# One more copy of v, a shorter warm-up, and five pooled normalisations moved to GpSimd, in a kernel of attention and two feed-forward layers

## The chip, the cores and the metric

The kernel runs on one core of one Trainium2 chip. The metric is the device time in microseconds (us) of one execution; the kernel before took 814.86 us in the median of three runs (814.63 to 815.61). The core has four compute engines that run side by side and wait for one another through semaphores: TensorE (PE in the profile; its weight loads are listed as PEld), VectorE (DVE), ScalarE (ACT) and GpSimd (POOL). SyncE (SP) only issues DMA transfers here. Each engine takes its instructions strictly in the order in which they were written, so an instruction that waits holds up all that stand behind it on its engine.

## The reference, cut to what matters

```
# q, k, v: (4 batches, 8 heads, 576 positions, 64)
q_d, k_d, v_d = mean over groups of 4 positions            # 144 pooled positions
out_d     = softmax(q_d k_d^T / 8) v_d, repeated 4 times   # pooled attention
out_local = softmax(q k^T / 8, only |i - j| < 4) v         # band attention
x = (out_up + out_local) as (2304 tokens, 512)
h = x @ w_in;  x = (h * sigmoid(h)) @ w_out                # w_in 512x2048, w_out 2048x512
h = x @ w_in2; x = (h * sigmoid(1.702 h)) @ w_out2
```

All of it is float32. Each softmax subtracts the row's maximum, takes the exponential and divides by the row's sum.

## The kernel before, in words

Host code only rearranges the inputs. On the core the program has two stages.

**The attention stage** handles 16 units, each a pair of heads of one batch (units 0 to 3 are batch 0, units 4 to 7 batch 1, and so on). Every engine walks the units in its own `body`, and the bodies are staggered by one unit: in the body of unit n, TensorE first makes the band scores of n (`sc`), then transposes the three groups of the finished band weights of unit n-1 (`pt<-ident,pband`), makes the pooled scores of n (`hp<-sums`), transposes the pooled weights of n-1 (`pt<-ident,pavg`) and multiplies both with v (`po`). VectorE (L1111) takes the band maximum (L1120), subtracts it (L1123), takes the pooled maximum (L1127), sums the band exponentials (L1133) and inverts the sum (`rcb`, L1137), sums q and k over groups of four for the next unit (L1108), inverts the pooled sum (`rca`, L1145) and writes the result of the unit before into `x` (L1153). ScalarE copies the transposed weights out of PSUM (L1027 for the three band groups, L1031 for each of the two pooled groups), takes the exponentials, and multiplies the pooled weights `pavg` by `rca` (`normalise`, L1081, three instructions per unit). GpSimd (L968) multiplies the band weights by `rcb` (L974), pools v by two additions (`vpair` L980, `vavg` L984), and then, for half a weight pair per unit, makes the sums of quarters of the first layer's w_in (`sum_weights`, L1004 to L1010).

A few steps of the feed-forward stage are fitted into the units, by the tables at L767 to L771, whose keys are units: `ROUNDED` and `ROUNDED_W` make ScalarE round a part of x or a batch of weights to the matmul's format, `RESTS` and `RESTS_W` make VectorE compute what the rounding left over (L257, L302), and `SUMMED` makes GpSimd take differences of quarters of x (L271), half of one each time.

SyncE loads, per unit, q and k three units ahead (L888), v for pooling (`vn`, one buffer, L891), the windows of v (`vwin`, two buffers, L895), and in every even unit a raw pair of w_in into `G` (`first_raw`, L114). The next `vn` is loaded only when GpSimd's `vpair` has read the one before (`v_half`).

**The feed-forward stage** works the two layers as products of 2x2 blocks with seven multiplications in place of eight, each as three float32r matmuls (rounded with rounded, rounded with rest, rest with rounded), for six blocks of 768 tokens. It runs from about 106 us to the end, and the change does not touch its code. Its first three products are issued by TensorE between the pooled product of unit 14 and the transposes of unit 15.

Before the first unit TensorE runs `WARM` matmuls of zeros into PSUM, and `IDLE` more after the scores of units 0 and 1 (`keep_warm`, L1296). The functions that the diff touches, and what calls them, with the line numbers of the profile:

## Time and profile before

| | |
|---|---|
| median of three runs | 814.86 us |
| the profiled execution's own time | 815.39 us |
| its span, first to last instruction | 813.6 us |
| span / rest of that execution | 813.6 / 1.8 us |
| PE busy | 801.9 us, 99% |
| DVE busy | 654.1 us, 80% |
| ACT busy | 538.8 us, 66% |
| POOL busy | 192.5 us, 24% |

The profile is of one execution. "Busy" is the time in which an engine had an instruction under way; TensorE's matmuls overlap one another, so that its ends are modelled. GpSimd's 24% is an average: nearly all of its work lies in the first 170 us, above all in the attention stage. The change touches only the first 113 us, so that stage has to be read unit by unit, and not by the shares of the whole span.

### The profile page before, as it was taken

The numbers are of one execution on the slowest core, as the hardware profiler recorded it, in microseconds if no ns is written. First come the engines' busy times: TensorE is split into PE (matmuls) and PEld (weight loads), VectorE is DVE, ScalarE is ACT, GpSimd is POOL, SyncE is SP. The second block draws the span as 40 slices with busy tenths as digits, with TensorE's granted clock in tenths as the row PEclk, the third lists the DMA queues.
The fourth block names the chain that finished last, engine by engine and source line by source line (L and its number), as shares of the span: only waits on it lengthen the run. The fifth ranks groups of instructions, "written<-read, shape, count | busy, mean of one in ns | idle before, by whom it ended". The sixth has DMA issues, their size and how long they took to land.

```text
span 813.6 us, 15682 instructions
## 1 busy us (share of the span) xinstructions
PE 801.9 (99%) x5800; PEld 776.5 (95%) x5800; DVE 654.1 (80%) x944; ACT 538.8 (66%) x865; POOL 192.5 (24%) x199
## 2 busy tenths in 40 slices
PE   9999899999999999999999999999999999999998
PEld 5777699999999999999999999999999999999998
DVE  7999889999998767998768888899655688555466
ACT  5889776578745677655678555677455687455773
POOL 5789786720045420235300000000000000000000
PEclk9999999999999999999999999999999999999999
DMA  7887668776868797677887777878887778877873
GB/s 241 230 253 226 162 198 276 256 284 218 287 209 275 262 322 249 210 264 252 277 292 249 231 253 253 270 234 272 283 289 253 266 252 265 301 251 262 279 254 137
DMA packets 98331, 205.42 MB, mean 252 GB/s; under 512 B 8432, under 2 KB 56048, under 8 KB 98256
## 3 DMA queue, kind: packets, MB, share of 16 engines
q1 hardware_dynamic: 98256, 204.42, 76.5%
q8 instruction: 47, 0.77, 0.4%
q14 instruction: 28, 0.23, 0.1%
HBM read 160.87 MB, written 43.52 MB: 251 GB/s over the span
## 4 chain that ended last, share of the span: by engine, by line
PE 81%; POOL 8%; DVE 7%; issue 4%; ACT 0%; POOLq 0%; DVEq 0%; ACTq 0%
PE hid L330 42%; PE yp L356 36%; DVE gr L547 2%; POOL vpair L980 2%; POOL pband L974 2%; DVE wh L302 2%; POOL vavg L984 1%; PE yp L372 1%; DVE xs L257 1%; POOL G L1005 1%; POOL G L1004 1%; POOL G L1008 1%; PE pt L1183 0%; POOL G L1010 0%; POOL x L271 0%
## 5 line engine op out<-in xcount | busy, mean ns | idle before, releaser
L330 PE MATMUL hid<-xs,wh 128*128 128x384 f32 x2016 | 351.5, 334 | 1.3 <-DVE hw L516 0.8
L330 PEld LDWEIGHTS hid<-xs,wh 128*128 128x128 f32 x2016 | 349.4, 188 | 2.5 <-issue 2.0
L356 PE MATMUL yp<-gr,wh 128*128 128x384 f32 x1968 | 342.1, 334 | 0.0
L356 PEld LDWEIGHTS yp<-gr,wh 128*128 128x128 f32 x1968 | 341.2, 188 | 0.0
L293 ACT ACTIVATE wh<-wr 128x1024 fp32r<-128x1024 f32 (+1 forms) x164 | 164.6, 1003 | 151.4 <-PE hid L330 121.3
L547 DVE TENSOR_TENSOR gr<-G,gr 128x768 fp32r<-128x768 f32 x144 | 137.9, 964 | 52.6 <-ACT gr L428 52.6
L428 ACT ACTIVATE gr<-G 128x768 fp32r<-128x768 f32 x144 | 121.8, 846 | 66.8 <-PE yp L356 66.8
L302 DVE TENSOR_TENSOR wh<-wr,wh 128x1024 fp32r<-128x1024 f32 x76 | 89.9, 1182 | 15.4 <-ACT wh L293 15.1
L391 ACT ACTIVATE G<-G 128x1152 f32<-128x1152 f32 x48 | 55.7, 1161 | 1.1 <-DVE G L542 1.1
L511 DVE TENSOR_TENSOR hv<-p,hid 128x384 f32<-128x384 f32 x48 | 26.3, 548 | 29.2 <-PE hid L330 29.2
L537 DVE TENSOR_TENSOR G<-hv,hid 128x384 f32<-128x384 f32 x48 | 26.4, 550 | 29.1 <-PE hid L330 28.8
L257 DVE TENSOR_TENSOR xs<-x,xs 128x768 fp32r<-128x768 f32 x42 | 42.4, 1011 | 0.0
L253 ACT ACTIVATE xs<-x 128x768 fp32r<-128x768 f32 x42 | 35.0, 833 | 1.5 <-POOL x L271 0.8
L479 DVE TENSOR_TENSOR G<-G 128x384 f32<-128x384 f32 x48 | 29.0, 604 | 7.5 <-ACT G L391 7.4
L630 POOL TENSOR_TENSOR G<-G 128x256 f32<-128x256 f32 x8 | 6.9, 862 | 103.1 <-DMA G<-in_w_in 52.3
L486 DVE TENSOR_TENSOR G<-G 128x384 f32<-128x384 f32 x48 | 28.5, 593 | 0.2
L539 DVE TENSOR_TENSOR gr<-G,gr 128x384 fp32r<-128x384 f32 x48 | 28.4, 593 | 0.0
L532 DVE TENSOR_TENSOR G<-hw,hid 128x384 f32<-128x384 f32 x48 | 26.4, 549 | 2.1 <-PE hid L330 1.6
L410 ACT ACTIVATE G<-hid 128x384 f32<-128x384 f32 x48 | 23.6, 493 | 6.0 <-PE hid L330 1.3
L516 DVE TENSOR_TENSOR hw<-hv,hid 128x384 f32<-128x384 f32 x48 | 26.3, 548 | 1.6 <-PE hid L330 1.2
L542 DVE TENSOR_TENSOR G<-hv,hid 128x384 f32<-128x384 f32 x48 | 26.4, 550 | 0.5
L293 ACT ACTIVATE wh<-G 128x1024 fp32r<-128x1024 f32 (+1 forms) x16 | 15.3, 955 | 17.3 <-PE hid L330 17.3
(101 smaller groups left out, 782.7 us busy)
## 6 DMA issues: line engine op xcount, KB each, us to landing
wh<-rests SPq DMA_DIRECT2D x72, 512.0 KB, 3.8
wr<-sums_out SPq DMA_DIRECT2D x48, 512.0 KB, 4.8
wr<-in_w_out SPq DMA_DIRECT2D x36, 512.0 KB, 5.4
rests<-wh SPq DMA_DIRECT2D x36, 512.0 KB, 3.4
wr<-sums_in SPq DMA_DIRECT2D x40, 384.0 KB, 4.0
wr<-in_w_in SPq DMA_DIRECT2D x40, 256.0 KB, 3.6
qk<-in_qkT SPq DMA_DIRECT2D x11, 576.0 KB, 7.1
G<-in_w_in SPq DMA_DIRECT2D x12, 512.0 KB, 5.5
```

Source lines behind the costliest of these rows:

```text
L253: eng.activation(xs[:, 0, q], features(n, q), ACT.Copy).then_inc(self.x_hi, 1)
L257: eng.tensor_tensor(xs[:, 1, q], features(n, q), xs[:, 0, q].bitcast(F32), ALU.subtract).then_inc(self.x_lo, 1)
L293: eng.activation(wh[:, w % SLOTS, 0, 0:entries(w), :], raw(w), ACT.Copy).then_inc(w_hi, 1)
L302: eng.tensor_tensor(wh[:, w % SLOTS, 1, 0:e, :], raw(w), wh[:, w % SLOTS, 0, 0:e, :].bitcast(F32), ALU.subtract).then_inc(w_lo, 1)
L330: last = eng.matmul(hid[:, at, 0:HALF], lhsT=wh[:, w % SLOTS, part, a % 4, cc * P:(cc + 1) * P], rhs=xs[:, rest, q, cc, :], start=start an ...
L356: last = eng.matmul(yp[:, at + m, 0:HALF], lhsT=wh[:, w % SLOTS, part, p % 4, m * P:(m + 1) * P], rhs=gr[:, p, rest, :], start=start and p ...
L391: eng.activation(G[:, s % PAIRS, G12:G22 + 1, :], G[:, s % PAIRS, G12:G22 + 1, :], ACT.Silu, scale=scale).then_inc(self.gate, 1)
L428: eng.activation(gr[:, 2 * a:2 * a + 2, 0, :], G[:, 2 * a:2 * a + 2, at, :], ACT.Copy).then_inc(self.g_hi, 1)
L479: eng.tensor_tensor(G[:, p, G11, :], G[:, p, G12, :], G[:, p, G11, :], ALU.subtract).then_inc(self.t_sum, 1)
L486: eng.tensor_tensor(G[:, p, G12, :], G[:, p, G22, :], G[:, p, G12, :], ALU.subtract).then_inc(self.t_sum, 1)
L539: eng.tensor_tensor(gr[:, p, 1, :], G[:, p, G11, :], gr[:, p, 0, :].bitcast(F32), ALU.subtract).then_inc(self.b11_lo, 1)
L547: eng.tensor_tensor(gr[:, 2 * a:2 * a + 2, 1, :], G[:, 2 * a:2 * a + 2, SECOND[i][1], :], gr[:, 2 * a:2 * a + 2, 0, :].bitcast(F32), ALU.s ...
```

## The change

It has six parts.

1. `vn` becomes two buffers, the second in the first 1024 columns of `yt`, which is idle in this stage. The load for unit n+2 is issued when unit n's `vpair` is done. The semaphores are split by buffer. The `vwin` load moves ahead of the wait for `v_half` on SyncE's queue.
2. `first_raw` is issued in odd units (and unit 0), each pair one unit sooner than before.
3. In units 1 to 5 (`POOLED`) GpSimd normalises the pooled weights with one `tensor_tensor` of 112x432 straight behind the band's; ScalarE leaves it out there.
4. `SUMMED` moves one unit sooner (6 to 13), `ROUNDED_W` from units 7, 10, 12 to 4, 6, 8.
5. ScalarE copies both pooled groups with one instruction of 72x672 in place of two of 72x336.
6. `WARM` goes from 11 to 8 matmuls, `IDLE` from (7, 6) to (4, 6).

```diff
-            vn = sb("vn", [HP, 2, FACTOR * 2 * D])[:]
+            vn = [sb("vn", [HP, 2, FACTOR * 2 * D])[:], ffn.yt[0:HP].rearrange("p a m n -> p (a m n)")[
+                :, 0:2 * FACTOR * 2 * D].rearrange("p (j n) -> p j n", j=2)]
...
-    ROUNDED_W = {7: 0, 10: 1, 12: 2}
+    ROUNDED_W = {4: 0, 6: 1, 8: 2}
+    POOLED = range(1, 6)
-    SUMMED = {7: (T1, 0), 8: (T1, 1), 9: (T3, 0), 10: (T3, 1), 11: (T2, 0), 12: (T2, 1), 13: (T4, 0), 14: (T4, 1)}
+    SUMMED = {6: (T1, 0), 7: (T1, 1), 8: (T3, 0), 9: (T3, 1), 10: (T2, 0), 11: (T2, 1), 12: (T4, 0), 13: (T4, 1)}
-    WARM = 11
-    IDLE = (7, 6)
+    WARM = 8
+    IDLE = (4, 6)
...
 # SyncE
             def start(u):
...
                 load_qk(u.after().after())
+                load_vn(u.after())
                 load_vwin(u.after())
...
-                if u.n + 1 < UNITS:
+                if u.n + 1 < UNITS and not first:
+                    eng.wait_ge(band_out, u.n)
+                    load_vwin(u.after())
+                if u.n + 2 < UNITS:
                     eng.wait_ge(v_half, u.n + 1)
-                    load_vn(u.after())
-                    if not first:
-                        eng.wait_ge(band_out, u.n)
-                        load_vwin(u.after())
-                if not u.odd:
+                    load_vn(u.after().after())
+                if first:
+                    ffn.first_raw(eng, 0)
+                elif u.odd and u.n + 1 < UNITS:
                     if u.half:
                         eng.wait_ge(ffn.w0_sum, 4 * u.half - 2)
-                    ffn.first_raw(eng, u.half)
+                    ffn.first_raw(eng, u.half + 1)
...
 # GpSimd, behind the band's normalisation
-                eng.wait_ge(vn_in, DMA_INC * (u.n + 1))
+                if u.n in POOLED:
+                    eng.wait_ge(a_rcp, u.n + 1)
+                    e = pavg[u.odd]
+                    eng.tensor_tensor(e[:], e[:], rca[:].unsqueeze(2).broadcast_to([AR, NA, SD]),
+                                      ALU.mult).then_inc(a_nrm, NA)
+                eng.wait_ge(vn_in[u.odd], DMA_INC * (u.half + 1))
...
 # ScalarE
-                else:
-                    eng.activation(pta[0:HP, j - NLG, :], pt[bank][0:HP, 0:NA * AR],
-                                   ACT.Copy).then_inc(p_cp, 1)
+                elif j == NG - 1:
+                    eng.activation(pta[0:HP], pt2[0:HP, :, 0:NA * AR], ACT.Copy).then_inc(p_cp, 2)
...
-                if last is not None and u.n:
+                if last is not None and u.n and u.n not in POOLED:
                     normalise(u)
```

How the program's order changes, at three places. First GpSimd's instructions in units 1 and 2, from the band's normalisation (`pband`) on; `G` is the sum of weights. Before:

```order
L974 TENSOR_TENSOR pband<-pband,rcb 128x9x70
L980 TENSOR_TENSOR vpair<-vn 72x512
L984 TENSOR_TENSOR vavg<-vpair 72x256
L1004 TENSOR_TENSOR G<-G 128x256
L1005 TENSOR_TENSOR G<-G 128x256
L974 TENSOR_TENSOR pband<-pband,rcb 128x9x70
L980 TENSOR_TENSOR vpair<-vn 72x512
```

and with the change:

```order
L982 TENSOR_TENSOR pband<-pband,rcb 128x9x70
L987 TENSOR_TENSOR pavg<-pavg,rca 112x432
L993 TENSOR_TENSOR vpair<-yt 72x512
L997 TENSOR_TENSOR vavg<-vpair 72x256
L1017 TENSOR_TENSOR G<-G 128x256
L1018 TENSOR_TENSOR G<-G 128x256
L982 TENSOR_TENSOR pband<-pband,rcb 128x9x70
L987 TENSOR_TENSOR pavg<-pavg,rca 112x432
L993 TENSOR_TENSOR vpair<-vn 72x512
```

The pooled weights stand ahead of v's pooling and of the sums of weights, all of which come later by that instruction and its wait for `rca`.

Second, GpSimd in units 6 and 7; `x<-x` is a difference of quarters of x. Before:

```order
L974 TENSOR_TENSOR pband<-pband,rcb 128x9x70
L980 TENSOR_TENSOR vpair<-vn 72x512
L984 TENSOR_TENSOR vavg<-vpair 72x256
L1008 TENSOR_TENSOR G<-G 128x256
L1010 TENSOR_TENSOR G<-G 128x256
L974 TENSOR_TENSOR pband<-pband,rcb 128x9x70
L980 TENSOR_TENSOR vpair<-vn 72x512
L984 TENSOR_TENSOR vavg<-vpair 72x256
L1004 TENSOR_TENSOR G<-G 128x256
L1005 TENSOR_TENSOR G<-G 128x256
L271 TENSOR_TENSOR x<-x 128x384
```

and with the change:

```order
L982 TENSOR_TENSOR pband<-pband,rcb 128x9x70
L993 TENSOR_TENSOR vpair<-vn 72x512
L997 TENSOR_TENSOR vavg<-vpair 72x256
L1021 TENSOR_TENSOR G<-G 128x256
L1023 TENSOR_TENSOR G<-G 128x256
L271 TENSOR_TENSOR x<-x 128x384
L982 TENSOR_TENSOR pband<-pband,rcb 128x9x70
L993 TENSOR_TENSOR vpair<-yt 72x512
L997 TENSOR_TENSOR vavg<-vpair 72x256
L1017 TENSOR_TENSOR G<-G 128x256
L1018 TENSOR_TENSOR G<-G 128x256
L271 TENSOR_TENSOR x<-x 128x384
```

Unit 6 has the difference of x already, ahead of the band's normalisation of unit 7.

Third, SyncE's queue of DMA issues from the bodies of units 0 to 3 (`qk`, and `wt` as the third of its buffers, is q and k; `G` a raw pair of weights; `vn` and `yt` are v). Before:

```order
L888 DMA qk<-in_qkT 128x1152
L891 DMA vn<-in_v 72x1024
L114 DMA G<-in_w_in 128x1024
L888 DMA qk<-in_qkT 128x1152
L891 DMA vn<-in_v 72x1024
L895 DMA vwin<-in_vw 70x1152
L888 DMA wt<-in_qkT 128x1152
L891 DMA vn<-in_v 72x1024
L895 DMA vwin<-in_vw 70x1152
L114 DMA G<-in_w_in 128x1024
```

and with the change:

```order
L892 DMA qk<-in_qkT 128x1152
L895 DMA vn<-in_v 72x1024
L114 DMA G<-in_w_in 128x1024
L892 DMA qk<-in_qkT 128x1152
L899 DMA vwin<-in_vw 70x1152
L895 DMA yt<-in_v 72x1024
L114 DMA G<-in_w_in 128x1024
L892 DMA wt<-in_qkT 128x1152
L899 DMA vwin<-in_vw 70x1152
L895 DMA vn<-in_v 72x1024
```

The second raw pair goes out ahead of the load of q and k of unit 5 instead of behind it, and each v is one unit further ahead of its use.

## Rows read from the trace of the kernel before

**Rows 1.** The page: the chain that ended last, share of the span by engine

```profile
PE 81%; POOL 8%; DVE 7%; issue 4%; ACT 0%; POOLq 0%; DVEq 0%; ACTq 0%
```

**Rows 2.** Windows: stretch, its length, then busy us (x instructions) per engine, clock, DMA

```profile
54.00:106.00 52.00, 46.26 (x848) 36.59 (x838) 45.77 (x89) 44.46 (x143) 46.28 (x48) 1.00 0.73 199
...
113.00:168.00 55.00, 55.00 (x319) 54.99 (x318) 52.15 (x78) 32.30 (x46) 36.94 (x36) 1.00 0.73 249
```

**Rows 3.** Timeline of PE: start, us, instruction, [idle before <- what ended it]

```profile
48.19 0.82 PE L1183 MATMUL pt<-ident,pband 128*70 128x128 f32 x6
...
54.19 0.85 PE L1183 MATMUL pt<-ident,pband 128*70 128x128 f32 x6
...
61.04 0.82 PE L1183 MATMUL pt<-ident,pband 128*70 128x128 f32 x6 [0.81 <-POOL pband L974]
...
93.71 0.82 PE L1183 MATMUL pt<-ident,pband 128*70 128x128 f32 x6 [0.94 <-POOL pband L974]
```

**Rows 4.** Timeline of PE at the program's start (L1299 is the warm-up)

```profile
3.96 0.63 PE L1299 MATMUL hp<-zeros 128*128 128x512 bf16 x1
4.38 0.53 PE L1299 MATMUL sc<-zeros 128*128 128x512 bf16 x1
...
4.97 0.38 PE L1299 MATMUL sc<-zeros 128*128 128x512 bf16 x1
5.19 0.43 PE L1194 MATMUL sc<-band,ident 128*128 128x350 bf16 x2
```

**Rows 5.** Timeline of DVE in unit 0

```profile
4.77 1.35 DVE L1108 TENSOR_REDUCE sums<-qk 128x288 f32<-128x1152 f32 x1 [0.60 <-DMA qk<-in_qkT]
6.80 0.88 DVE L1120 TENSOR_REDUCE mxb<-sc 128x5 f32<-128x350 f32 x2 [0.68 <-PE sc L1201]
```

**Rows 6.** Waits of POOL from 16 to 113 us: total us, times, longest

```profile
POOL vpair L980 <- DMA vn<-in_v: 1.4, 2, 1.2
POOL G L1004 <- DMA G<-in_w_in: 1.1, 2, 0.7
```

**Rows 7.** Timeline of POOL, units 5 to 8 and 12 to 14

```profile
40.03 1.24 POOL L974 TENSOR_TENSOR pband<-pband,rcb 128x630 f32<-128x630 f32 x1 [0.81 <-DVE rcb L1137]
...
46.80 1.24 POOL L974 TENSOR_TENSOR pband<-pband,rcb 128x630 f32<-128x630 f32 x1 [2.12 <-DVE rcb L1137]
...
52.39 1.24 POOL L974 TENSOR_TENSOR pband<-pband,rcb 128x630 f32<-128x630 f32 x1 [0.82 <-DVE rcb L1137]
...
56.78 1.83 POOL L1005 TENSOR_TENSOR G<-G 128x256 f32<-128x256 f32 x1
...
59.65 1.24 POOL L974 TENSOR_TENSOR pband<-pband,rcb 128x630 f32<-128x630 f32 x1
...
87.85 1.26 POOL L980 TENSOR_TENSOR vpair<-vn 72x512 f32<-72x512 f32 x1 [1.22 <-DMA vn<-in_v]
...
92.33 1.24 POOL L974 TENSOR_TENSOR pband<-pband,rcb 128x630 f32<-128x630 f32 x1
...
96.25 0.72 POOL L1005 TENSOR_TENSOR G<-G 128x256 f32<-128x256 f32 x1
96.94 0.99 POOL L271 TENSOR_TENSOR x<-x 128x384 f32<-128x384 f32 x1
...
99.87 1.24 POOL L974 TENSOR_TENSOR pband<-pband,rcb 128x630 f32<-128x630 f32 x1 [1.94 <-DVE rcb L1137]
```

**Rows 8.** Timeline of ACT: the pooled normalisation of unit 1

```profile
17.32 1.02 ACT L1081 ACTIVATE pavg<-pavg,rca 112x144 f32<-112x144 f32 x3 [0.52 <-DVE rca L1145]
```

**Rows 9.** Timeline of DVE: the rests of units 6, 8, 14

```profile
44.80 0.95 DVE L257 TENSOR_TENSOR xs<-x,xs 128x768 fp32r<-128x768 f32 x1
...
56.81 1.22 DVE L302 TENSOR_TENSOR wh<-G,wh 128x1024 fp32r<-128x1024 f32 x1
...
96.30 2.44 DVE L257 TENSOR_TENSOR xs<-x,xs 128x768 fp32r<-128x768 f32 x1
...
99.51 0.21 DVE L1137 RECIPROCAL rcb<-smb 128x9 f32<-128x9 f32 x1
```

More of the change, by code:

```diff
@@ L91, in __init__ @@
         self.wh = keep("wh", [P, self.SLOTS, 2, 4, 256], F32R)
-        self.w0_in, self.w0_sum = sem("w0_in"), sem("w0_sum")
+        self.w0_in, self.w0_sum = [sem(f"w0_in{i}") for i in range(2)], sem("w0_sum")
         self.w0_out = [sem(f"w0_out{p}") for p in range(self.PAIRS)]
@@ L115, in first_raw @@
                              self.w_in[0][bass.ds(p, 1)].rearrange("a p n -> (a p) n")).then_inc(
-                                 self.w0_in, DMA_INC)
+                                 self.w0_in[p % 2], DMA_INC)
     def first_place(self, p, a):
@@ L856, in build @@
         vwin_in = [sem(f"vwin_in{i}") for i in range(2)]
-        vn_in = sem("vn_in")
+        vn_in = [sem(f"vn_in{i}") for i in range(2)]
         qk_in = [sem(f"qk_in{i}") for i in range(3)]
@@ L890, in load_vn @@
             def load_vn(u):
-                eng.dma_start(vn, v[bass.ds(u.n, 1), :, :].rearrange(
-                    "a (p j r) d -> (a p) j (r d)", j=2, r=FACTOR)).then_inc(vn_in, DMA_INC)
+                eng.dma_start(vn[u.odd], v[bass.ds(u.n, 1), :, :].rearrange(
+                    "a (p j r) d -> (a p) j (r d)", j=2, r=FACTOR)).then_inc(vn_in[u.odd], DMA_INC)
             def load_vwin(u):
@@ L936, in _ @@
                 eng.wait_ge(band_out, UNITS)
+                eng.wait_ge(v_half, UNITS)
                 ffn.load_pair(eng, q)
@@ L975, in body @@
                                   ALU.mult).then_inc(b_nrm, 1)
-                eng.wait_ge(vn_in, DMA_INC * (u.n + 1))
+                if u.n in POOLED:
[4 more added lines that the diff above has]
+                eng.wait_ge(vn_in[u.odd], DMA_INC * (u.half + 1))
                 if not first:
                     eng.wait_ge(v_sum, u.n)
-                rows = vn.rearrange("p j (r d) -> p r j d", r=FACTOR)
+                rows = vn[u.odd].rearrange("p j (r d) -> p r j d", r=FACTOR)
                 eng.tensor_tensor(vpair[:], rows[:, 0:2], rows[:, 2:4], ALU.add).then_inc(v_half, 1)
@@ L1002, in sum_weights @@
                 if u.odd:
-                    eng.wait_ge(ffn.w0_in, DMA_INC * (p + 1))
+                    eng.wait_ge(ffn.w0_in[p % 2], DMA_INC * (p // 2 + 1))
                     eng.tensor_tensor(at(S1), at(A21), at(A22), ALU.add).then_inc(ffn.w0_sum, 1)
```

## The prediction, on record before the changed kernel ran

> **What bounds the kernel now.** The first view is the chain of waits that ended last: TensorE holds 81% of it, GpSimd 8%, VectorE 7% [rows 1]. 8% of 813.6 us is 65 us of GpSimd, an engine with only 192.5 us of work in all, so the second view is the busy time by stretch. From 113 us on TensorE is busy 55.00 of 55 us [rows 2]: the feed-forward stage goes at TensorE's own pace, the change doesn't touch its code, and whatever is gained or lost before 113 us is carried to the end as it is. From 54 to 106 us GpSimd is busy 46.28 of 52 us, as much as TensorE's 46.26 and VectorE's 45.77. There no engine's share says who is waited for, so the third view is TensorE's timeline, at the transposes of the band weights of each unit, which need GpSimd's normalisation.
>
> Two regimes show. Up to unit 7 TensorE has no gap: from the transposes of unit 6 to those of unit 7 it needs 54.19 - 48.19 = 6.00 us [rows 3]. From unit 8 it waits for GpSimd's `pband`: 0.81 us in unit 8, 0.94 in unit 13 [rows 3]. GpSimd's own timeline tells why. In units 5 to 7 it still idles before `pband` (0.81, 2.12, 0.82 us), in unit 8 no more [rows 7]: from unit 7 on the extra 0.99 us of `x<-x` fills its unit, and in every second unit a VectorE rest that runs beside it stretches one of its instructions from 0.73 to 1.83 us [rows 7]. And in this regime it waits for transfers, 1.4 us for v and 1.1 us for raw weights, two times each [rows 6]; the longest is 1.22 us at 87.85 [rows 7]. These 2.5 us stand in a queue without slack.
>
> **The two v buffers and the sooner raw weights.** They add no transfer. v is asked for a whole unit (5.6 us at least) sooner, and the wait of 1.22 us is far shorter; the raw weights, with waits up to 0.7, likewise. I take all 2.5 us away from GpSimd. SyncE stands behind `v_half` as before, now one pooled normalisation later in five units; q and k, behind it, are loaded three units ahead, so I price that at nothing. The one new transfer at the start, v of unit 1, goes out behind q, k and v of unit 0 and delays nothing that unit 0 waits for.
>
> **The pooled normalisation.** ScalarE gives up 1.02 us in five units [rows 8]. What is late there is not ScalarE but TensorE at 6.00 us per unit, so the gain is nothing. The cost is on GpSimd. The trace has no such instruction. From below, the broadcast product of 630 elements takes 1.24 us [rows 7], by elements 432/630 x 1.24 = 0.85. From above, the plain one of 384 takes 0.99, so 432/384 x 0.99 = 1.11. It broadcasts like the first, with a fixed part: I take 0.95. In front of it GpSimd waits for `rca`: the band product starts 0.36 us after `rcb` (99.87 against 99.51 [rows 7, 9]) and takes 1.24, and ScalarE, which waits for `rca`, started at 17.32 in unit 1 [rows 8]; that is estimated at 0.2 us behind the band product. So 1.15 us per unit, 0.3 more or less for all bounds, pushed onto `vpair`, `vavg` and the sums.
>
> The cover is GpSimd's idle time. Unit 5 had 0.81 before `pband` [rows 7]: 1.15 - 0.81 = 0.35 late, ending at 41.6, and TensorE comes for it about 42.2, so hidden. In unit 6 the cover breaks. GpSimd was idle from 44.68 (46.80 - 2.12); VectorE's rest started at 44.80 [rows 9] and met nobody. Now GpSimd works to 44.68 + 0.35 + 1.15 = 46.2, beside that rest, and is stretched by some 0.95 (1.83 - 0.73 = 1.1 at the longer rest of 56.81): 47.1 instead of 46.80, and TensorE 0.3 us late. Its first difference of x then comes in unit 6 too: a back-to-back unit with it is 5.7 us, so `pband` of unit 7 is at 47.1 + 5.7 = 52.8 instead of 52.39, 0.4 late, and TensorE (48.5 + 6.0) doesn't see it.
>
> **From unit 8 on.** `pband` of unit 8: 59.65 + 0.4, less the wait for raw weights in unit 7 (0.4, the shorter of the two) = 59.65, no gain yet. From there to unit 13 the other waits go: 2.5 - 0.4 = 2.1, so 92.33 - 2.1 = 90.2 [rows 7]. TensorE's own cycle of nearly 6.0 gives about 0.2 of that back in unit 13: its transposes at 91.8 instead of 93.71 [rows 3], 1.9 gained.
>
> Unit 14 held one more loss. VectorE's rest at 96.30 took 2.44 us for 0.95: it started beside GpSimd's pair of 96.25 and 96.94 and ended 0.8 us after that pair was through at 97.93 [rows 7, 9]. The same rest now comes at 91.8 + (96.30 - 93.71) = 94.4, and GpSimd works to 90.2 + 5.6 = 95.8. Held to the end again, it is over at 96.7, and `rcb` at 97.5 instead of 99.51: 2.0 gained. Not held, as those of 44.80 and 56.81 weren't (0.95 and 1.22 us), GpSimd is stretched instead to 96.8, against `pband` at 99.87 before: 3.0 gained. I take 2.5. Behind it the chain to the first feed-forward product runs as before.
>
> The Trainium skill (GPSIMD Engine Reference, section Key points) says that GpSimd shares its SBUF interfaces with VectorE and contends with VectorE instructions that have two SBUF inputs. That speaks against a change that gives GpSimd more to do. The trace agrees at 56.78 and 96.30 [rows 7, 9]; who yields the rule doesn't say, and on that hangs the first rival below.
>
> **The sooner roundings, the one copy, fewer warm-up matmuls.** Roundings of weights move into units where ScalarE has room; GpSimd's difference is now a unit ahead, so ScalarE's rounding never waits for it. Nothing on the path. One copy of 672 for two of 336 reads as many elements; a fixed part of at most 0.1 us goes, off TensorE's path: nothing. If the copy had to wait for its second half, 0.1 to 0.3 us at the last unit alone.
>
> The warm-up ends the start of the band scores: they begin at 5.19, right behind the eleventh [rows 4], while q and k had landed by 4.77, where VectorE ends a 0.60 us wait for them. VectorE waits 0.68 us for those scores at 6.80 [rows 5]. Eight matmuls end about 4.4, so the landing is next: 5.19 - 4.77 = 0.4 us gained, nothing to 0.45 at the bounds. It shifts everything behind it.
>
> **The sum.** 0.4 (start) + 2.5 (through unit 14) = 2.9, less 0.3 for rests that may now be held in units 4 to 12, where GpSimd has become busier: 2.6 us. The profiled execution took 815.39 us, so 812.8 by it; it was 0.5 above the median, so the median goes from 814.86 to 812.3. What a measurement of this kernel tells from no change is about 0.2%, 1.6 us.
>
> **Rivals.**
> *Held rests.* This is the way to slower. GpSimd now runs beside the rests of units 4 and 6 too, and keeps running beside those of 8, 10, 12. For it: 96.30, 1.5 us lost. Against: of four rests beside GpSimd in the loop one was held, and 56.81 is among the three that weren't. A held rest in units 8 to 12 puts `pband` at GpSimd's end + 0.9 (the rest) + 0.8 (98.74, its end, to `rcb` at 99.51) + 0.3 instead of GpSimd's end + 1.0: 1.0 us each. In unit 6 1.1 beyond the forecast, in unit 4 0.7 after TensorE's slack. All five 4.8; with unit 14 held too (0.5), 2.9 - 5.3 = -2.4: 817.3 us. It is slower than before from the third of the five on.
> *Two or so held.* The same mechanism, as often as the old trace had it: unit 14 held and one or two others, 2.9 - 0.5 - 1.0 to 2.0: 812.5 + 1.4 = 813.9 us. What was gained in waits is handed back to the shared port.
> *A late clock.* TensorE's warm-up matmuls stand 0.42 us apart at 3.96 and 0.22 at 4.97 [rows 4], so 1.2 GHz and then 2.4 GHz, the change at about 4.7. With eight, TensorE falls idle from 4.4 to 4.8, just there. If the clock then rises only later, the band scores, 1.6 us from 5.19 to 6.80, take 3.2: end at 8.0, 1.6 later than forecast. Against it: 3.4 us of unbroken work lie before the gap, which is short. 812.3 + 1.6 = 813.9 us. The Trainium skill (TensorE: Matmul & The Clock Gate, Part 1: The HAM clock gate) says the gate judges recent busyness on a beat of its own that no kernel start resets; by that the rise could fall anywhere near here in both kernels and differ between executions.
> *The transfers stay late.* Sooner issues could only crowd the DMA engines (share 0.73 from 54 to 106 [rows 2]). If only half of the 2.1 us went: 812.3 + 1.0 = 813.3.
>
> **Chances.** Forecast 0.55, two or so held 0.17, late clock 0.11, transfers late 0.11, held rests 0.06. The forecast's own range is 811.2 to 813.1: the ends of unit 14 (0.5 each way) with those of the pooled product and the start. Over all cases 810.8 to 815.2. Faster by over 0.2% means below 813.2: nearly all of the forecast, and half of the transfers' case: 0.64. Slower by over 0.2% is above 816.5: 0.05. The rest, 0.31, is within.
>
> **What would show it.** Right: no `vpair` or `G` wait for a DMA behind unit 1; band scores of unit 0 at 4.8; the pooled product 0.85 to 1.11 us; transposes of units 2 to 7 still 6.0 us apart, minus 0.4; those of unit 13 near 91.4; the first feed-forward product 2 to 3.5 us sooner. Wrong: rests of 1.8 us or more in several units; matmuls of the first band scores at twice their spacing; DMA waits that are still there; or a feed-forward stage that no longer takes the same time, since I let nothing change there.

## The result, and the profile after

The changed kernel takes 820.2 us in the median of 9 runs (817.58 to 826.08), the kernel before 814.86 beside it; the ratio is 1.0062, with an interval of 1.0045 to 1.008. It is slower, by some 5 us, where 2.6 us of gain were forecast. The profiled execution took 817.58 us (span 815.8), the mildest of the nine, 2.2 above the profiled one of before; it shows the kinds of loss, not their whole size.

First the part that came as forecast. The waits of GpSimd from 16 to 113 us (total us, times, longest):

```profile
POOL pband L982 <- DVE rcb L1150: 10.9, 6, 3.5
POOL pavg L987 <- DVE rca L1158: 1.0, 3, 0.3
```

The waits for v and for raw weights [rows 6] are gone. The new product, by its line:

```profile
L987 POOL TENSOR_TENSOR pavg<-pavg,rca x5: 906/906/906, 18.4 to 42.8; 112x432 f32<-112x432 f32 x5
```

But one of the six waits for `rcb` is 3.5 us long. The waits of TensorE over the attention stage, 13 to 113 us, first of the kernel before:

```profile
PE pt L1183 <- POOL pband L974: 5.1, 5, 1.5
PE hid L330 <- issue: 0.4, 1, 0.4
PE pt L1183 <- issue: 0.4, 1, 0.4
```

and of the changed kernel:

```profile
PE hp L1237 <- issue: 2.1, 1, 2.1
PE pt L1196 <- POOL pband L982: 1.2, 4, 0.7
PE sc L1214 <- issue: 1.1, 3, 0.5
PE hid L330 <- issue: 0.4, 1, 0.4
```

TensorE waits for GpSimd 1.2 us in place of 5.1, which is what the change could win. In its place stand waits with the releaser "issue": the view names nothing that the engine waited for. The longest is inside a group of matmuls that needs nothing from another engine. TensorE's timeline there (start, us, instruction, [idle before <- what ended it]):

```profile
81.26 0.85 PE L1196 MATMUL pt<-ident,pband 128*70 128x128 f32 x6
81.94 0.49 PE L1196 MATMUL hp<-ident,pband 128*70 128x128 f32 x3
82.37 0.44 PE L1237 MATMUL hp<-sums 64*48 64x144 f32 x2
84.89 1.35 PE L1237 MATMUL hp<-sums 64*48 64x144 f32 x10 [2.08 <-issue]
86.17 1.34 PE L1196 MATMUL pt<-ident,pavg 112*72 112x112 f32 x6
87.45 1.80 PE L1266 MATMUL po<-yt,vwin 128*64 128x64 f32 x36
89.09 0.71 PE L1277 MATMUL po<-pta,vavg 128*64 128x144 f32 x8
```

Two of the twelve pooled-score matmuls are done, then 2.08 us of nothing, then the other ten, slower: the pooled transposes take 1.34 us here and 0.80 a unit later, the products with `vwin` 1.80 and 1.27. So one stall costs twice, once in itself and once in the clock behind it. VectorE's pooled maximum waits 2.76 us for these scores, GpSimd's `pband` behind it 3.48, and the transposes of unit 13 come at 97.20 instead of 93.71 [rows 3].

The stretches, by busy time (length, busy us per engine, granted clock, DMA share, GB/s); the first two answer to [rows 2]:

```profile
54.00:106.00 52.00, 47.40 (x823) 36.75 (x822) 44.98 (x89) 41.35 (x124) 43.22 (x46) 0.97 0.89 221
113.00:168.00 55.00, 55.00 (x354) 54.47 (x353) 51.02 (x77) 32.11 (x48) 37.88 (x36) 1.00 0.68 232
...
13.00:54.00 41.00, 40.33 (x729) 31.95 (x727) 37.05 (x75) 32.90 (x101) 36.60 (x39) 1.00 0.93 245
54.00:86.00 32.00, 28.27 (x495) 21.71 (x493) 26.79 (x54) 25.42 (x75) 28.75 (x30) 0.99 0.94 225
86.00:106.00 20.00, 19.13 (x330) 15.04 (x329) 18.20 (x35) 15.93 (x49) 14.47 (x16) 0.93 0.80 214
```

The same three stretches of the kernel before:

```profile
13.00:54.00 41.00, 40.20 (x754) 31.79 (x754) 37.32 (x77) 36.47 (x119) 30.02 (x34) 1.00 0.81 236
54.00:86.00 32.00, 29.87 (x559) 23.52 (x549) 29.52 (x59) 28.72 (x92) 29.83 (x30) 1.00 0.85 238
86.00:106.00 20.00, 16.38 (x289) 13.07 (x289) 16.24 (x31) 15.74 (x52) 16.45 (x19) 1.00 0.53 137
```

From 113 us on TensorE is full as before: nothing changed there. Ahead of it the DMA engines are busy 0.93 and 0.94 of the time in place of 0.81 and 0.85, while they move 245 and 225 GB/s in place of 236 and 238. The last stretch is 0.80 instead of 0.53, and the clock 0.93 instead of 1.00.

The 8 us just ahead of the stall show what a much higher share at nearly the same rate means: the DMA engines' busy tenths, the packets by queue and share of the engines' time, and the landing time of the load of q and k. Before, 73 to 81 us:

```profile
DMA  6994775141000091057999979969999957998899
...
q1 hardware_dynamic: 444, 1.69, 75.2%
q8 instruction: 1, 0.02, 0.7%
...
wt<-in_qkT SPq DMA_DIRECT2D x1, 576.0 KB, 8.3
```

After, the same stretch:

```profile
DMA  9999977999969959494893789997999699999699
...
q1 hardware_dynamic: 477, 1.82, 96.0%
...
wt<-in_qkT SPq DMA_DIRECT2D x1, 576.0 KB, 12.0
```

Before, the transfers pause: the row has several zeros. After, no slice falls under 3 tenths, 7% more packets take 28% more engine time, and the load lands after 12.0 us instead of 8.3. Over the whole stage q and k landed after 3.9/7.1/8.4 us (least, median, most) before and after 3.9/8.1/13.4 now. One more kind of packet uses the same DMA engines. Two lines of the changed kernel's page:

```profile
PE 805.0 (99%) x5794; PEld 778.4 (95%) x5794; DVE 651.9 (80%) x944; ACT 533.8 (65%) x834; POOL 195.5 (24%) x204
q8 instruction: 47, 0.77, 0.4%
```

The trace has 5794 matmuls, 5794 weight loads and 402 other instructions of TensorE, nearly all of them waits for a semaphore, 11,990 in all, and the 47 packets of queue q8 have 16 KB each: one packet for every 255 or 256 of its instructions. So q8 brings TensorE's own instructions. No q8 packet starts between 72.10 and 82.05 us, and the stall begins at 82.81. A long gap alone means little, since the kernel before has two of over 10 us between starts in this stage (the others are 5.4 to 8.0); what counts is when TensorE needs the packet, and the trace shows that too.

**Each stall stands at a packet's edge.** Number TensorE's instructions in the trace in their order, from 0, and take each q8 packet with its start and end (no view lists them singly; what follows is counted from the trace's records). The three longest stalls of the changed kernel ahead of its first feed-forward product stand at the numbers 1986, 2242 and 2754, which are 194 and a multiple of 256. Call these places marks. Of 37 idle times of 0.25 us or more that all 16 traces of this document have with the releaser "issue" (13 us to the first feed-forward product), 30 stand at a mark, within one instruction, and end 1.3 to 1.8 us after a q8 packet has ended. Some of them (us; the last three rows are runs told below):

| kernel | q8 packet | stall | number | stall's end after the packet's |
|---|---|---|---|---|
| changed | 65.60 to 66.74 | 67.78 to 68.32 | 2242 | 1.58 |
| changed | 82.05 to 83.35 | 82.81 to 84.89 | 2754 | 1.54 |
| changed, long warm-up | 84.12 to 85.44 | 84.20 to 86.99 | 2755 | 1.55 |
| loads alone | 82.06 to 83.42 | 82.98 to 84.98 | 2755 | 1.56 |
| windows behind v | 51.67 to 52.77 | 52.92 to 54.17 | 1730 | 1.40 |

The other seven stand in front of the first product with `vwin`, and are waits for its load (see *More traffic*). At the twelve marks from 17 us on, in all 16 traces, TensorE never passes mark n before the n-th q8 packet has ended, and never less than 1.17 us after. So TensorE stops at a mark when the packet with its next instructions is late. How late packets come is seen from TensorE's passing of one mark to the start of the next packet: 3.0 us in the median before (5.1 at most), 3.8 in the changed kernel (7.1 at most).

Second, the start. TensorE's timeline, to be held against [rows 4]:

```profile
3.96 0.63 PE L1312 MATMUL hp<-zeros 128*128 128x512 bf16 x1
4.86 0.68 PE L1207 MATMUL sc<-band,ident 128*128 128x350 bf16 x2 [0.27 <-DMA qk<-in_qkT]
5.47 1.86 PE L1214 MATMUL sc<-qk 64*64 64x70 f32 x35
7.03 0.44 PE L1237 MATMUL hp<-sums 64*48 64x144 f32 x1
...
10.34 0.43 PE L1207 MATMUL sc<-band,ident 128*128 128x350 bf16 x2
```

The scores start at 4.86, as forecast, but at the low clock: the two of the band take 0.68 us, and 0.43 for those of unit 1. The first transposes come at 13.15 us; before they came at 11.96. From there to the transposes of unit 7 (55.30) the units are 6.0 us long as before. Against the kernel before, the profiled execution thus lost 1.2 us at the start, 0.8 in unit 9 and 2.7 in unit 12 (9.98 us from one unit's transposes to the next, 7.28 before). It won 1.0 in unit 13 and 0.8 in unit 14. The first feed-forward product is at 108.84 instead of 106.15.

### The profile page after: what moved, and what is told of

Its sections match the earlier page's. It is cut to its first block, busy times and chain, and to the rows that moved or that the text cites. A ratio compares the mean times of both kernels' runs of the same rounds, so it can differ in the third digit from the quotient of the medians.

```text
span 815.8 us, 15667 instructions
## 1 busy us (share of the span) xinstructions
PE 805.0 (99%) x5794; PEld 778.4 (95%) x5794; DVE 651.9 (80%) x944; ACT 533.8 (65%) x834; POOL 195.5 (24%) x204
## 4 chain that ended last, share of the span: by engine, by line
PE 87%; DVE 6%; POOL 3%; issue 3%; DMA 0%; ACT 0%; POOLq 0%; DVEq 0%; ACTq 0%
PE hid L330 42%; PE yp L356 36%; DVE gr L547 2%; PE pt L1196 2%; DVE wh L302 2%; PE po L1266 1%; PE hp L1237 1%; PE sc L1214 1%; PE yp L372 1%; POOL vpair L993 1%; DVE xs L257 1%; POOL pband L982 1%; PE po L1277 1%; DMA qk<-in_qkT 0%; POOL vavg L997 0%
## 5 line engine op out<-in xcount | busy, mean ns | idle before, releaser
L537 DVE TENSOR_TENSOR G<-hv,hid 128x384 f32<-128x384 f32 x48 | 26.4, 551 | 27.8 <-PE hid L330 27.6
L479 DVE TENSOR_TENSOR G<-G 128x384 f32<-128x384 f32 x48 | 27.3, 568 | 8.1 <-ACT G L391 8.1
L486 DVE TENSOR_TENSOR G<-G 128x384 f32<-128x384 f32 x48 | 27.8, 579 | 0.2
L630 POOL TENSOR_TENSOR wt<-wt 128x256 f32<-128x256 f32 x12 | 10.0, 836 | 70.6 <-DMA wt<-in_w_out 39.4
```

Source lines behind the costliest of these rows:

```text
L479: eng.tensor_tensor(G[:, p, G11, :], G[:, p, G12, :], G[:, p, G11, :], ALU.subtract).then_inc(self.t_sum, 1)
L486: eng.tensor_tensor(G[:, p, G12, :], G[:, p, G22, :], G[:, p, G12, :], ALU.subtract).then_inc(self.t_sum, 1)
```

## The experiments

The theory of the transfers (F in the expectations): the loads, more closely queued, make TensorE's instructions come late, and the stalls and low clock are the loss. The first rival (G): GpSimd's added work, which holds VectorE's rests. The second (W): the shorter warm-up. Each run was measured beside the kernel before on the same chip, and the chips differ between groups of runs: there the kernel before has medians of 815.7 to 816.2 us, not 814.86. So the ratios compare, and times of different groups only to about 1 us. "Stall" is an idle time of TensorE with the releaser "issue"; where it is a wait for `vwin` after all, the text says so.

### First, the parts in their groups

**The changed kernel with the long warm-up.**

```diff
-    WARM = 8
-    IDLE = (4, 6)
+    WARM = 11
+    IDLE = (7, 6)
```

> The changed kernel with the old warm-up (11 matmuls, idle 7 and 6). Theory F (fetch): the denser transfers starve TensorE's instruction fetch; it stalls inside a group of matmuls, where nothing is waited for, and its clock falls afterwards. Then this gives back only the late clock of the start, 1.0 to 1.5 us: 818.5 to 819.5 us, still with stalls inside groups between 55 and 106 us, still slower than before. Theory W (warm-up): the late clock is all of it; then about 814 us or below. Theory G (GpSimd's load): 818 to 819 us, but with held rests and late band normalisations in units 4 to 12 rather than stalls inside groups.

Measured: 821.15 us, ratio 1.0057 (1.0032 to 1.0082). The loss is all there (more than the 818.5 to 819.5 of theory F), so the short warm-up isn't its cause. Its trace has 7.3 us of stalls ahead of the feed-forward stage, the longest 2.8, and a clock of 0.83 from 86 to 106 us.

**The loads alone**, on the kernel before: v in two places, `vwin` ahead of v, raw weights a unit sooner (the SyncE part of the diff above), with the warm-up, the tables and the pooled normalisation as before.

> Of the change only the two places for v, the sooner raw weights and the sooner window load; old warm-up, old tables, no pooled normalisation on GpSimd, two copies. Theory F: the DMA share from 57 to 86 us rises from 0.84 to 0.94 as in the changed kernel, TensorE stalls inside groups, and the time is 815.5 to 819 us. Theory G: faster than before by the 2 us of DMA waits that GpSimd no longer has, 812 to 813. Theory W: the same, 812 to 814.

Measured: 820.5 us, 1.0043 (1.0012 to 1.0074). The loss is here, somewhat above theory F's range. TensorE in its trace has the same picture at nearly the same place, now in front of the transposes that go into `hp`:

```profile
84.98 0.49 PE L1196 MATMUL hp<-ident,pband 128*70 128x128 f32 x3 [2.00 <-issue]
85.40 1.68 PE L1237 MATMUL hp<-sums 64*48 64x144 f32 x12
87.01 1.35 PE L1196 MATMUL pt<-ident,pavg 112*72 112x112 f32 x6
```

The twelve pooled scores take 1.68 us, 0.94 at the high clock. The place agrees with the packets: this kernel has six more warm-up matmuls, twelve instructions with their weight loads, so the same mark falls twelve instructions sooner in the program.

**GpSimd's part alone**: `POOLED`, the sooner `SUMMED` and `ROUNDED_W`, the one copy; loads and warm-up as before.

> Of the change only the five pooled normalisations on GpSimd, the sooner tables and the one copy; v, raw weights and warm-up as before. Theory F: no stall inside groups or at most a short one, 813.5 to 815.5 us. Theory G: slower than before, 816 to 819, with rests of VectorE over 1.4 us in units 4 and 6. Theory W: 814 to 815.5.

Measured: 817.24 us, 1.0004 (0.9978 to 1.003). The DMA share is that of before (0.80, 0.80, 0.55 in the three stretches). But rests of VectorE are held here, as the rival *Held rests* had it:

```profile
57.44 2.71 DVE L302 TENSOR_TENSOR wh<-G,wh 128x1024 fp32r<-128x1024 f32 x1
```

This one took 1.22 us before [rows 9], and another took 2.45; they are those of units 8 and 12, not 4 and 6. That mechanism is real, and yet no loss shows that is clear of the interval, which reaches up to 2.4 us. GpSimd's work isn't the cause of the 5 us; *The swap, by itself* below shows the same, with all of that work and no loss.

**The short warm-up alone**, on the kernel before.

> Of the change only the shorter warm-up (8, and idle 4 and 6). Theory W: 818 us or more. Theories F and G: the clock rises at about 10 us instead of 4.7, the transposes of unit 0 come 1.0 to 1.3 us later than the 11.96 of before, and the time is 815.5 to 816.3 us, without a stall inside a group.

Measured: 817.01 us, 0.9998 (0.9975 to 1.002). No effect that can be measured, and the late start that theories F and G expected isn't in its trace: the first transposes came at 12.01. The trace shows something else. With the loads of the kernel before, GpSimd waits 8.1 us for v and 2.5 for raw weights here, where the trace of before has 1.4 and 1.1 [rows 6]: the price of these waits, on which the forecast rests, varies much from one execution to another.

### Which of the loads

**v in two places alone** (`load_vn(u.after().after())`), `vwin` behind it and the raw weights as before.

> The kernel before with v in two places alone (v for unit n+2 asked for when unit n is pooled; windows of v behind it and raw weights as before). Theory F, version v: the load of v at this moment is what crowds the transfers; DMA share from 57 to 86 us above 0.90, stalls inside groups, time above that of before by 2 us or more. If the windows' place is what crowds them: share 0.84 as before, no long stall, and the time of before or 1 us less. Theory G (GpSimd bound) expects 1 to 2 us less.

Measured: 816.07 us, 0.9999 (0.9976 to 1.0022). The DMA share is 0.89, 0.76 and 0.73 in the three stretches, and one stall of 0.58 us is in the trace, so this place alone doesn't crowd the transfers. GpSimd waits for no v, but 7.4 us for raw weights, and the gain of 1 to 2 us that theory G expected isn't there either.

**`vwin` ahead of the wait for `v_half` alone**, v in one place.

```diff
+                if u.n + 1 < UNITS and not first:
+                    eng.wait_ge(band_out, u.n)
+                    load_vwin(u.after())
                 if u.n + 1 < UNITS:
                     eng.wait_ge(v_half, u.n + 1)
                     load_vn(u.after())
-                    if not first: ...
```

> The kernel before with the windows of v asked for ahead of v (as soon as the band product of the unit before is done) and nothing else: one buffer for v. Theory F, version windows: transfers spread over the whole unit instead of one burst, DMA share from 57 to 86 us above 0.90, stalls inside groups, 2 us or more above before. Otherwise as before within 1 us.

Measured: 816.62 us, 1.0008 (0.9994 to 1.0022). The share is 0.78, 0.76 and 0.61, and no stall reaches 0.3 us. GpSimd still waits 8.7 us for v.

**The raw weights a unit sooner alone** (the `first_raw` lines of the diff).

> The kernel before with the raw weights asked for a unit sooner and nothing else. Theory F in both versions: DMA share and time as before (within 1 us), since the same bytes go out in odd units instead of even ones; GpSimd's waits for them (1.1 us in all) gone. If this alone crowds the transfers: share above 0.90 and 2 us or more above before.

Measured: 815.27 us, 0.9984 (0.9972 to 0.9996): faster by 1.3 us, and the only single part of the change that shows an effect, just clear of its interval. Its trace has 2.5 us of stalls, none over 1.0, and 7.9 us in which GpSimd waits for v. None of the three alone has the loss.

**More traffic**: the kernel before, and in each unit from the second on one more load of 288 KB of v into a place that nobody reads.

```diff
+                if u.n:
+                    if u.n > 1:
+                        eng.wait_ge(more_in, DMA_INC * (u.n - 1))
+                    eng.dma_start(<1024 columns of yt>, v[...]).then_inc(more_in, DMA_INC)
```

> The kernel before with one more load of v per unit, 288 KB into a buffer that nobody reads; nothing waits for it but SyncE and the first load of the next stage. Theory F: more transfers alone, at no change of any engine's work, must bring the stalls inside groups and the fall of the clock: 3 to 10 us above before, DMA share near 1. Theories G and W: no more than 1 us above before, or waits for late q, k or v by an engine, which the trace would name.

Measured: 837.36 us (5 runs), 1.0254 (1.0235 to 1.0273), 21 us slower, where theory F had 3 to 10. TensorE in one of five places with the releaser "issue":

```profile
42.34 2.19 PE L1261 MATMUL po<-yt,vwin 128*64 128x64 f32 x36 [2.11 <-issue]
44.29 1.18 PE L1272 MATMUL po<-pta,vavg 128*64 128x144 f32 x8
```

These look like the stalls above, 5.5 us in all, but four of the five are none. They stand at no mark, and in front of the first product with `vwin`, where TensorE's semaphore instruction waits for the load of `vwin` and a copy of ScalarE (its duration, least, median and most in ns, from 20 to 113 us here, then over the changed kernel's whole trace):

```profile
L1258 PEldq EVENT_SEMAPHORE  x12: 601/2107/3238, 25.3 to 112.7; - x12
L1263 PEldq EVENT_SEMAPHORE  x16: 51/51/208, 14.8 to 113.6; - x16
```

The load that this product needed landed at 42.25 us, and the product began at 42.34. With four more idle times of this kind, which the view puts down to ScalarE, TensorE waits 9.2 us for windows. One stall of 0.61 us is at a mark. Behind the two longest waits (2.11 and 1.99 us) the clock is the low one (1.18 us for the eight, else 0.71), behind the other three it isn't. GpSimd waits 16.8 us for v and 14.3 for raw weights. So this dose shows that load on the DMA engines makes data late, for TensorE too. It doesn't show the stalls of the changed kernel: TensorE, held elsewhere, reaches its marks late enough, although the packets start 5.2 us after the mark before, in the median.

### Less traffic, and the pairs

**Less traffic**: the changed kernel whole, short warm-up too, with v loaded for units 0 and 1 alone. Later units pool the v of these two, so their pooled attention is of the wrong v, and GpSimd waits for the first two loads alone; 14 loads of 288 KB are left out. From 13 to 113 us that is 15% of the bytes (21.45 to 18.30 MB), not a fifth.

```diff
                 if u.n + 2 < UNITS:
                     eng.wait_ge(v_half, u.n + 1)
-                    load_vn(u.after().after())
```

> The changed kernel as it is, warm-up too, but v for pooling is loaded for units 0 and 1 only (later units pool those again, so their pooled attention is computed from the wrong v): 14 loads of 288 KB, a fifth of the stage's traffic, are left out, and no engine's work changes. Theory F: loads of q and k land in 8 us or less again, no stall of TensorE inside a group over 0.6 us, no fall of the clock in the stage, and the time is what the prediction had for the engines' work, 811.5 to 814 us, 6 us or more under the changed kernel. Theory G: 817 us or more still, since GpSimd and VectorE have the same work in the same order.

Measured: 811.96 us (811.31 to 813.58, 9 runs), 0.9959 (0.9943 to 0.9974). By the ratios that is 3.3 us under the kernel before and some 8 us under the changed kernel. The stretches of before, again:

```profile
13.00:54.00 41.00, 40.01 (x754) 31.67 (x750) 37.32 (x76) 32.23 (x100) 36.89 (x39) 1.00 0.69 220
54.00:86.00 32.00, 30.15 (x559) 23.84 (x551) 29.76 (x60) 28.05 (x86) 31.30 (x31) 1.00 0.60 199
86.00:106.00 20.00, 19.16 (x306) 15.86 (x304) 17.63 (x35) 18.88 (x54) 18.80 (x19) 1.00 0.36 115
```

The clock is 1.00 throughout, q and k land after 5.5 us in the median, a q8 packet starts 1.5 us after the mark before it (3.7 at most), and no stall is over 0.3 us. TensorE at the places that the forecast named:

```profile
91.59 0.85 PE L1195 MATMUL pt<-ident,pband 128*70 128x128 f32 x6
...
102.82 1.45 PE L330 MATMUL hid<-xs,wh 128*128 128x384 f32 x7 [0.28 <-issue]
```

91.59 for unit 13, where the forecast had 91.4, and 102.82 for the first feed-forward product, 3.3 us sooner than before, where it had 2 to 3.5. GpSimd waited for no v in the changed kernel either, so what the missing loads take away is load on the DMA engines, and not a wait for v. But the share is also far under that of the kernel before (0.81 and 0.85), and no run leaves the same loads out of the kernel before. How much of the 3.3 us is the engines' accounting and how much is the lighter traffic isn't shown.

**GpSimd's part with the sooner raw weights**; v, windows and warm-up as before.

> The kernel before with the pooled normalisations, the sooner tables, the one copy and the sooner raw weights, and with v, its windows and the warm-up as before. Theory F: transfers no denser than in e3 and e7, no long stall; 0 to 2 us under before, 814 to 816 on this chip. Theory G: 1 us or more above before.

Measured: 815.76 us, 1.0001 (0.9986 to 1.0016). The longest stall is 0.85 us.

**The windows behind v**: the changed kernel with the order of the two loads as before, and the long warm-up.

```diff
-                if u.n + 1 < UNITS and not first:
-                    eng.wait_ge(band_out, u.n)
-                    load_vwin(u.after())
                 if u.n + 2 < UNITS:
                     eng.wait_ge(v_half, u.n + 1)
                     load_vn(u.after().after())
+                if u.n + 1 < UNITS and not first:
+                    eng.wait_ge(band_out, u.n)
+                    load_vwin(u.after())
```

> The changed kernel with the old warm-up and one swap on SyncE's queue: the windows of v behind v again. If the windows' sooner place is needed to crowd the transfers: 4 us or more under e1, 814 to 816.5 us, landings of q and k 8 us or less in the median. If v in two places with sooner raw weights crowds them by itself: 819 to 822 as e1.

Measured: 813.6 us (811.28 to 819.58), 0.9987 (0.9967 to 1.0006). The loss is gone with the swap undone. The share falls to 0.89, 0.82 and 0.71, q and k land after 6.8 us in the median, a q8 packet starts 2.3 us after the mark before it; one stall of 1.25 us is left, at a mark. Its start has eleven warm-up matmuls and a late clock all the same:

```profile
5.24 0.63 PE L1312 MATMUL sc<-zeros 128*128 128x512 bf16 x1
5.67 0.73 PE L1207 MATMUL sc<-band,ident 128*128 128x350 bf16 x2
```

**v in two places with the windows ahead**, all else as before, the raw weights too: the same two parts from the other side.

> The kernel before with v in two places and the windows of v ahead of it, raw weights as before (e2 without the raw weights). If these two together take the pause out of the transfers: 819 to 821 us as e2, q and k landing in about 10 us. If it needs the sooner raw weights too: 815.5 to 817, 8 us.

Measured: 821.75 us (6 runs), 1.0079 (1.0048 to 1.011), with 2.5 us of stalls at marks (q and k land after 8.2 us, not 10), the longest:

```profile
34.39 0.77 PE L1194 MATMUL pt<-ident,pavg 112*72 112x112 f32 x6 [1.43 <-issue]
```

Alone the two parts cost nothing that could be measured (0.9999 and 1.0008), together 6 us. Not all of that need be stalls: GpSimd waits 4.3 us for raw weights in this trace.

### The swap, by itself

**The changed kernel with the swap undone and the short warm-up kept**: the edit of the windows behind v, with `WARM = 8`.

> The changed kernel with one swap alone: the windows of v behind v again; the short warm-up stays. If the transfers' order is the whole cause: 813 to 814.5 us, below before, and 6 us or more below the changed kernel. If the short warm-up costs: 1 us or more above e11's 813.6. The clock's rise should fall anywhere between 4 and 10 us, as in the kernels with the long one.

Measured: 814.3 us, 0.9988 (0.997 to 1.0006). One swap of two loads on SyncE's queue thus takes the changed kernel from a ratio of 1.0062 to 0.9988, some 6 us, and the warm-up makes no difference that shows (0.9987 with the long one). The profiled execution was one of the slowest of its twelve (819.75) and shows that stalls are not gone. Two of them, of 1.42 and 1.45 us, stand at marks. A longer idle time is no stall:

```profile
85.66 0.80 PE L1196 MATMUL pt<-ident,pavg 112*72 112x112 f32 x6
88.82 1.27 PE L1266 MATMUL po<-yt,vwin 128*64 128x64 f32 x36 [2.35 <-issue]
```

The semaphore instruction in front of these products took 3.49 us (window 85 to 89 us):

```profile
L1263 PEldq EVENT_SEMAPHORE  x1: 3494/3494/3494, 85.3 to 85.3; - x1
```

It ended with the load of `vwin`, asked for at 83.95 and landed at 88.73. So the order of before has a price too: the windows are asked for late, and where the transfers are crowded (a DMA share of 0.91, 0.93 and 0.74 in this execution) TensorE waits for them, 4.2 us in three places. In the traces of *The windows behind v* and of the next run no idle time of 0.25 us or more has this cause. The products behind this one take the 1.27 us of the high clock: 2.35 us of idle time didn't bring the low one.

**The windows behind v, with raw weights as before**: the long warm-up too.

> e11 with the raw weights asked for in even units as before. If the sooner raw weights carry a part of the gain: 0.5 to 1.5 us above e13. If they crowd the transfers: below e13 and with a narrower spread.

Measured: 816.44 us, 1.0008 (0.9992 to 1.0024), against 0.9987 with the sooner raw weights. It looks as if they carried what is gained, as when alone, but the intervals overlap, and GpSimd's part with them shows 1.0001: that isn't shown.

## Why the prediction was wrong

**The failed step** is this: "They add no transfer." and, of SyncE and of q and k behind it, "I price that at nothing". It is true that nothing is added. But the loads were spaced by their waits, and the change takes two spacers away: v needs no longer wait for its own buffer's reader, and `vwin` no longer stands behind `v_half`. Together they close the pauses of the transfers (share 0.81 and 0.85 to 0.93 and 0.94) and cost 6 us; each alone leaves a spacer and costs nothing that could be measured. Undoing one of them, in the changed kernel, gives the 6 us back. The sum has no term for what the closer transfers do to TensorE: it put at nothing what came out as 2.08 us in one stall, with a low clock behind it.

**The rival that came nearest** was that the transfers stay late, priced at +1.0 with a chance of 0.11. It had the share of 0.73 in hand and asked the wrong question: it counted what GpSimd would lose in waits for data, and GpSimd's waits for data all went. The price fell on TensorE, which in the changed kernel's trace waits for no transfer of data in this stage (the semaphore instruction for `vwin` takes 0.2 us at most), but for transfers of its own instructions. No rival had that form, and the range ended at 815.2.

**What lies between share and stall.** That a stall is TensorE without its next instructions is shown by the marks: 30 stalls in 13 traces at the same place of every 256 instructions, each ending 1.3 to 1.8 us behind a q8 packet, and no mark passed without its packet. That these packets are late because data packets keep the same engines busy is shown in the tendency: from one mark to the start of the next packet it is 1.5 us in the median with less traffic, 3.0 in the kernel before, and 3.8, 4.9 and 4.5 in the changed kernel, with the long warm-up and with the loads alone. Executions scatter around it (1.6 and 2.0 in two kernels at a share of 0.76 to 0.79), and what a packet waits behind, no row shows.

**The terms that held.** The pooled product took 0.906 us (forecast 0.95) and waited at most 0.3 us for `rca`. It was hidden but for unit 6, where TensorE waited 0.16 us (forecast 0.3). The DMA waits of GpSimd went, 2.5 us. With the traffic lowered the time is 811.96, against 812.3, and unit 13 comes at 91.59, against 91.4. That agrees with the accounting of the engines, but the closeness is partly luck: by the ratio the gain was 3.3 us and not 2.6, the traffic was lighter than before too, and the 2.5 us of waits are one execution's (10.6 in the trace with the short warm-up alone). What the accounting was made for, TensorE's 5.1 us of waiting for `pband`, did go down to 1.2 in the changed kernel.

**The held rests.** Forecast as a cost of 0.3; no run measures it by itself. In the changed kernel the rests took 0.95 to 1.22 us but for two of 1.53 and 1.66; with GpSimd's part alone two took 2.45 and 2.71. The Trainium skill (GPSIMD Engine Reference, section Key points) says that GpSimd shares its SBUF interfaces with VectorE and contends with VectorE instructions that have two SBUF inputs; the trace agrees, and shows that either may yield: at 45.67 a sum of GpSimd took 1.60 us in place of 0.73 beside a rest that kept its 0.95.

**The start.** 0.4 us were forecast. The profiled execution lost 1.2 to a late clock, which was a rival for 0.11. But over the runs this isn't the change's doing. With eight warm-up matmuls the first transposes came at 11.73, 11.87, 12.01 and 13.15 us in four profiled executions; with eleven, in twelve, between 11.62 and 13.06, four of them at 12.81 or later. Both warm-ups give early and late starts, and the two comparisons (alone 0.9998; 0.9988 against 0.9987) show nothing. The one rise of the clock as late as 10.2 us is the changed kernel's; with eleven the latest of twelve is 7.0, so a rarely later rise with fewer isn't ruled out. The Trainium skill (TensorE: Matmul & The Clock Gate, Part 1: The HAM clock gate) says that no kernel start resets the gate's beat, and these spreads agree. The scores do start sooner (4.86), but that gains nothing on average that could be measured: the 0.4 us of the sum aren't shown by any comparison.

**What stays open.** What a late instruction packet waits behind; how the 5 us divide into stalls, low clock and what follows on the other engines, since the one trace of the changed kernel is its mildest execution; what decides, in one kernel, between an execution with few stalls and one with many; and whether either version with the windows behind v is truly faster than before. Their ratios are 0.9987 and 0.9988, and both intervals reach 1.0006.

## What to carry to other kernels

A wait that spaces transfers is doing work, even where no engine waits for what is behind it: before taking two such waits away, look at the pauses in the DMA row and ask what else uses those engines, the instructions of the fullest engine first. Read TensorE's idle times with the releaser "issue" with care. In the middle of a group, at a constant place of every 256 instructions and just behind an instruction packet, it is late instructions. In front of a group that has a semaphore instruction, look at that instruction's duration first: here seven such idle times were late loads. And a bundle of parts that are each neutral need not be neutral: here two cost 6 us only together.

## What the runs showed of the hardware

- TensorE's instructions came in packets of 16 KB through the DMA engines while the kernel ran, 47 packets for its 11,990 instructions. Where one was late TensorE stood still at the packet's edge, 30 times in 13 traces, and went on 1.3 to 1.8 us after it had ended.
- These stalls lasted 1.1 to 2.8 us at a time only in stretches with a DMA share of 0.75 or more (not in each such: the kernel before has none at 0.85), and at most 0.3 us at 0.60 to 0.69. After stalls of 2.0 and 2.1 us the clock fell (six transposes 1.34 us instead of 0.80); after one of 1.45, and after a wait of 2.35, it didn't. The clock of 54 to 86 us was 0.95 in the short warm-up alone and in `vwin` ahead alone too, where no idle time named "issue" in this stage is over 0.42 us, but TensorE waits 5.6 and 5.0 us for `pband`: a fall needs no stall.
- The same load of 576 KB landed after 5.5 us in the median at a share of 0.60 to 0.69, 7.1 at 0.81 to 0.85, 8.1 and 10.3 at 0.93 to 0.94 (the changed kernel and the loads alone), and 10.1 with the added traffic. In the 8 us ahead of the stall the packets' engine time was 28% more for 7% more packets.
- The clock at the program's start rose 4.0 to 7.0 us after the first instruction in twelve executions with eleven warm-up matmuls, and at 4.3, 5.3, 5.8 and 10.2 us in four with eight.
- A product of 112x432 with a broadcast factor on GpSimd took 0.906 us, five times out of five.
- Where GpSimd and VectorE overlapped, either was stretched: a sum of 128x256 on GpSimd to 1.60 us for 0.73, a VectorE rest to 2.71 for 1.22.
